# A gated-recurrence, token-mixing and gating kernel in one launch: one decay scan over all head pairs, key and query scaling on VectorE, token weights split in place by output half

## What is computed

```python
# block 1: gated linear attention, state (B, H, 48, 48)
for t in range(S):
    state = alpha[:, :, t, :, None] * state + einsum('bhd,bhe->bhde', k[:, :, t], v[:, :, t])
    y[:, :, t] = einsum('bhd,bhde->bhe', q[:, :, t], state)
# block 2, x = y as (B, S, 384)
theta = x @ w_theta
zr, zi = x * cos(theta), x * sin(theta)
y = einsum('ts,bsd->btd', w_tok_r, zr) + einsum('ts,bsd->btd', w_tok_i, zi)
u = x + y
x2 = u + maximum(u @ w_ch, 0)
# block 3
h = maximum(x2 @ w_in, 0); u, v = h[..., :512], h[..., 512:]
v_n = (v - mean(v)) / sqrt(var(v) + 1e-6)
out = (u * (einsum('ts,bsd->btd', w_spatial, v_n) + b_spatial)) @ w_out
```

## Time and profile before

| | us |
|---|---|
| median of 3 runs | 657.05 (651.57 to 658.28) |
| the profiled execution | 655.44 |
| its span, first to last instruction | 653.6 |
| PE busy | 603.7 (92%) |
| DVE busy | 408.4 (62%) |
| POOL busy | 247.4 (38%) |
| ACT busy | 224.1 (34%) |
| DMA queue of the program | 48.77 MB |
| mean granted TensorE clock | 0.963 of full speed |

### The profile page before, as it was taken

One profiled execution on the slowest core, in us unless ns is written; L12 is line 12 of the kernel. 1 busy time (PEld: TensorE's weight loads), 2 busy tenths in 40 slices (PEclk: granted clock), 3 DMA queues, 4 the chain that ended last, 5 costly groups with the idle time before them and its releaser, 6 DMA issues.

```text
span 653.6 us, 11285 instructions
## 1 busy us (share of the span) xinstructions
PE 603.7 (92%) x4608; PEld 568.1 (87%) x4608; DVE 408.4 (62%) x733; ACT 224.1 (34%) x410; POOL 247.4 (38%) x205
## 2 busy tenths in 40 slices
...
GB/s 333 164 119 109 62 62 60 62 62 97 69 55 158 62 93 66 62 155 65 50 48 105 102 48 314 2 73 0 38 36 73 1 62 12 1 1 74 0 1 73
DMA packets 18580, 49.49 MB, mean 76 GB/s; under 512 B 1632, under 2 KB 12128, under 8 KB 18016
## 3 DMA queue, kind: packets, MB, share of 16 engines
q1 hardware_dynamic: 18528, 48.77, 21.6%
...
## 4 chain that ended last, share of the span: by engine, by line
PE 61%; DVE 21%; ACT 6%; issue 5%; DMA 4%; POOL 3%; ACTq 0%; DVEq 0%
PE psY L388 10%; PE psS L487 8%; PE psF L487 8%; PE psC L370 5%; DVE akq L723 4%; PE psS L465 4%; DVE after L711 4%; PE psF L455 4%; PE psF L475 4%; PE psS L475 3%; PE psF L465 3%; DVE total L715 3%; PE psC L405 3%; PE psS L321 2%; PE psF L349 2%
## 5 line engine op out<-in xcount | busy, mean ns | idle before, releaser
L923 POOL TENSOR_TENSOR z_lo<-cos_sin,z_hi 128x768 fp32r<-128x768 f32 x24 | 46.4, 1935 | 137.0 <-ACT z_hi L579 137.0
L983 POOL TENSOR_TENSOR gated_lo<-u_gated,gated_hi 128x384 fp32r<-128x384 f32 x32 | 32.4, 1013 | 124.3 <-ACT gated_hi L675 124.2
L723 DVE TENSOR_TENSOR_SCAN akq<-akq,rtotal,zeros 128x128 f32<-128x128 f32 x96 | 56.4, 646 | 0.6
L388 PE MATMUL psY<-tok_r_hi,z_hi 128*128 128x384 f32 x144 | 52.9, 367 | 3.5 <-POOL z_lo L923 3.3
L711 DVE TENSOR_TENSOR_SCAN after<-akq,zeros 128x127 f32<-128x127 f32 x96 | 45.9, 539 | 8.8 <-DMA akq<-akq 8.8
L349 PE MATMUL psF<-v,scores 128*64 128x48 f32 x768 | 39.4, 232 | 11.1 <-issue 10.7
L388 PE MATMUL psY<-tok_i_hi,z_hi 128*128 128x384 f32 x144 | 49.1, 341 | 0.0
L388 PE MATMUL psY<-tok_r_hi,z_lo 128*128 128x384 f32 x144 | 49.1, 341 | 0.0
L388 PE MATMUL psY<-tok_i_lo,z_hi 128*128 128x384 f32 x144 | 49.0, 340 | 0.0
L388 PE MATMUL psY<-tok_r_lo,z_hi 128*128 128x384 f32 x144 | 48.9, 340 | 0.0
L388 PE MATMUL psY<-tok_i_hi,z_lo 128*128 128x384 f32 x144 | 48.8, 339 | 0.0
...
## 6 DMA issues: line engine op xcount, KB each, us to landing
...
```

Of the source, the lines that this page charges most:

```text
L388: mm = pe.matmul(psY[:, j, 0:HALF], Z[s][l][:, q, tile(j)], W[m][:, s, half(h)], start=(s == 0 and q == 0 and n == 0), stop=(s == CHUNKS - ...
L723: op = dve.tensor_tensor_scan(AKQ[s][:, 0, p, :], AKQ[s][:, 0, p, :], zeros[:], rtotal[:, s, p:p + 1], ALU.mult, ALU.add)
L923: pool.tensor_tensor(Z[c][1][:], trigs[g % 2][:], f(Z[c][0][:]), ALU.subtract).then_inc(z_lo, 1)
L983: pool.tensor_tensor(GA[1][:, j, half(h)], ug[h][:, j], f(GA[0][:, j, half(h)]), ALU.subtract).then_inc(g_lo, 1)
```

## The change

- **One scan.** The decays get a 129th column per head pair that holds 0, so that one scan over 516 columns passes from pair to pair: the tile `restart` puts a 1 there (backwards), and `rtotal`, now 517 columns with the reciprocals at every 129th, puts the pair's reciprocal there (forwards). The product over all 128 decays then stands in column 0 of each pair of `after`, so that the multiply for `total` is gone. There is one `after` instead of two.
- **Scaling on VectorE.** POOL's `scale_keys` and `scale_queries` are gone; DVE multiplies k right behind the reciprocal and q right behind the second scan.
- **Order.** In the first six chunks DVE runs `mask_scores(c)` ahead of `decay_keys(c + 1)`, and `reduce_angle(c - 1)` ahead of `decay_queries(c + 1)`; ACT runs `xT_high(c)` ahead of `sines(c - 1)`.
- **Weights.** Raw weights are loaded into the place of their low part and split there. A piece is now two row blocks by one output half (384 columns), 12 pieces as before and as large as before. `SPLITS` says behind which chunk a piece is split: the last four behind chunks 6 and 7. `w_ch` is split in chunk 4. PE's wait for everything ahead of chunk 6 is gone; it waits for the pieces of a unit, and for `ch_lo` at the first `channel_mix` (chunk 7).
- **Loads.** The decays of chunk 0 are a DMA of their own, `w_theta` is loaded ahead of chunk 1, six pieces follow, the other six behind `load_chunk(3)`.

```diff
+SEG = P + 1
+SCAN = PAIRS * SEG
+SPLITS = ((0, 1), (2, 3), (4,), (5,), (), (6, 7), (8, 9), (10, 11)) + ((),) * (BATCH * CHUNKS)
...
+        def tok_part(i):
+
+            h, rest = divmod(i, CHUNKS)
+            pair, m = divmod(rest, 2)
+            return m, slice(2 * pair, 2 * pair + 2), half(h)
...
@@ sync
             load_chunk(0)
+            sp.dma_start(raw_theta[:], w_theta.rearrange("(c p) n -> p c n", p=P)).then_inc(theta_in, 16)
             load_chunk(1)
-            sp.dma_start(raw_theta[:], w_theta.rearrange("(c p) n -> p c n", p=P)).then_inc(theta_in, 16)
-            for i in range(RAWS):
+            for i in range(CHUNKS):
                 load_tok(i)
+            load_chunk(2)
             sp.dma_start(raw_ch[:], w_ch.rearrange("(c p) n -> p c n", p=P)).then_inc(ch_in, 16)
-            for c in range(3):
-                load_chunk(2 + c)
-                load_tok(RAWS + 2 * c)
-                load_tok(RAWS + 2 * c + 1)
+            load_chunk(3)
+            for i in range(CHUNKS):
+                load_tok(CHUNKS + i)
+            load_chunk(4)
             load_chunk(5)
@@ tensor
-                if k == 0:
-                    pe.wait_ge(tok_lo, 2 * s + 2)
+                if k < HALVES:
+                    pe.wait_ge(tok_lo, k * CHUNKS + s // 2 * 2 + 2)
...
+                if n == 0:
+                    pe.wait_ge(ch_lo, 1)
...
             angles(CHUNKS - 1, 0)
-            pe.wait_ge(ch_lo, 1)
-            pe.wait_ge(tok_lo, 2 * CHUNKS)
@@ scalar
                 copy_x(c)
+                xT_high(c)
                 if c:
                     sines(c - 1)
-                xT_high(c)
                 keep_xT(c)
                 if c:
                     z_high(c - 1)
-                tok_high(2 * c)
-                tok_high(2 * c + 1)
-            act.wait_ge(ch_in, 16)
-            act.activation(WC[0][:], raw_ch[:], ACT.Copy).then_inc(ch_hi, 1)
+                if c == CHUNKS - 2:
+                    act.wait_ge(ch_in, 16)
+                    act.activation(WC[0][:], raw_ch[:], ACT.Copy).then_inc(ch_hi, 1)
+                for i in SPLITS[c]:
+                    tok_high(i)
@@ vector
-                for p in range(PAIRS):
-                    op = dve.tensor_tensor_scan(after[s][:, p, P - 2::-1], AKQ[s][:, 0, p, P - 1:0:-1],
-                                                zeros[:, 0:P - 1], 1.0, ALU.mult, ALU.add)
-                op.then_inc(after_made, 1)
+                dve.tensor_tensor_scan(after[:, ::-1], ALPHA[s][:, ::-1], restart[:, ::-1], 1.0,
+                                       ALU.mult, ALU.add).then_inc(after_made, 1)
                 dve.wait_ge(after_made, g + 1)
-                dve.tensor_tensor(total[:, s, :], after[s][:, :, 0], AKQ[s][:, 0, :, 0], ALU.mult).then_inc(total_made, 1)
-                dve.wait_ge(total_made, g + 1)
-                dve.reciprocal(rtotal[:, s, :], total[:, s, :]).then_inc(rtotal_made, 1)
+                need(dve, decayed, g)
+                dve.reciprocal(rtotal[:, 0:SCAN:SEG], AFTER[:, :, 0]).then_inc(rtotal_made, 1)
+                if g == 0:
+                    dve.wait_ge(akq_in[0], 16)
+                dve.tensor_tensor(K[s], K[s], AFTER[:, :, 1:SEG], ALU.mult).then_inc(k_scaled, 1)
...
-                for p in range(PAIRS):
-                    op = dve.tensor_tensor_scan(AKQ[s][:, 0, p, :], AKQ[s][:, 0, p, :], zeros[:],
-                                                rtotal[:, s, p:p + 1], ALU.mult, ALU.add)
-                op.then_inc(decayed, 1)
+                dve.tensor_tensor_scan(ALPHA[s], ALPHA[s], rtotal[:, 1:], rtotal[:, 0:1],
+                                       ALU.mult, ALU.add).then_inc(decayed, 1)
+                dve.wait_ge(decayed, g + 1)
+                dve.tensor_tensor(Q[s], Q[s], ALPHA[s].rearrange("p (q t) -> p q t", q=PAIRS)[:, :, 0:P],
+                                  ALU.mult).then_inc(q_scaled, 1)
...
             for c in range(CHUNKS):
+                mask_scores(c)
                 decay_keys(c + 1)
-                mask_scores(c)
-                decay_queries(c + 1)
                 if c:
                     reduce_angle(c - 1)
+                decay_queries(c + 1)
                 update_state(c)
@@ gpsimd
-            def scale_keys(g):
-                pool.wait_ge(after_made, g + 1)
-                pool.tensor_tensor(AKQ[g % 2][:, 1], AKQ[g % 2][:, 1], after[g % 2][:], ALU.mult).then_inc(k_scaled, 1)
-
-            def scale_queries(g):
-                pool.wait_ge(decayed, g + 1)
-                pool.tensor_tensor(AKQ[g % 2][:, 2], AKQ[g % 2][:, 2], AKQ[g % 2][:, 0], ALU.mult).then_inc(q_scaled, 1)
...
             for c in range(CHUNKS):
-                scale_keys(c + 1)
-                scale_queries(c + 1)
                 if c:
                     z_low(c - 1)
-                tok_low(2 * c)
-                tok_low(2 * c + 1)
-            pool.wait_ge(ch_hi, 1)
-            pool.tensor_tensor(WC[1][:], raw_ch[:], f(WC[0][:]), ALU.subtract).then_inc(ch_lo, 1)
+                if c == CHUNKS - 2:
+                    pool.wait_ge(ch_hi, 1)
+                    pool.tensor_tensor(WC[1][:], raw_ch[:], f(WC[0][:]), ALU.subtract).then_inc(ch_lo, 1)
+                for i in SPLITS[c]:
+                    tok_low(i)
```

More of the change, by code:

```diff
@@ L108, in build @@
         work_at = r.offset
-        AKQ = [r(f"akq{i}", [3, PAIRS, P]) for i in range(2)]
+        AKQ = [r(f"akq{i}", [SCAN + 2 * PAIRS * P]) for i in range(2)]
         late_at = r.offset
-        after = [r(f"after{i}", [PAIRS, P]) for i in range(2)]
+        after = r("after", [SCAN])
         V = [r(f"v{i}", [D]) for i in range(2)]
```

118 lines of the change are left out of this document (63 added, 55 removed).

## The result

| | us |
|---|---|
| changed kernel, median of 4 runs | 635.13 (634.82 to 635.71) |
| before, 4 runs on the same chip | 655.87 (651.57 to 658.28) |
| ratio, 95% interval | 0.9692 [0.9638, 0.9746] |
| profiled execution's span, before and after | 653.6, 633.0 |

The change saves 20.7 us; the profiled spans differ by 20.6. The forecast was 645.0, a saving of 11.3 in the profile.

What follows compares the result with a forecast made beforehand. PE bounds 115.14 to 350.00 us; in early chunks DVE waits for POOL, and PE idles ahead of chunk 6. Terms -1.8 - 1.8 + 0.3 - 1.5 - 8.0 + 0.6 + 0.9 = -11.3 from 655.44; forecast 645.0 us, range 637 to 652.

Steps and rivals of the forecast that it cites:

- the start: Start and chunks 0 and 1: chunk 0's scores start earlier and `update_state(1)` ends at 29.1 instead of 30.9, -1.8 us.
- chunk 5 with the gate: Chunk 5's angles no longer wait for `xT_lo`, -1.5 us; PE's wait ahead of chunk 6 goes, -7.96 us.
- rival 3: Steady chunks: a long scan costs far more than four short ones; loses from 1.86 us, up to 664 us; chance 0.07.
- Rival 1: Only removing PE's wait ahead of chunk 6 pays, early chunks keep their 15 us: 647.4 us; chance 0.19.
- Rival 4: Chunks 6 to 8 give back 4 to 6 us more, the last pieces sharing POOL: about 650 us; chance 0.11.
- Rival 2: Early chunks gain more if the clock stays at 2.4 GHz: chunk 4 some 14 us, about 639 us; chance 0.13.
- Chunk 2: DVE's chain meets POOL's work, the scan just missing the door: 14.9 us against 14.5 before.
- Chunk 4: PE's own 16.7 us, which it keeps, as DVE's lead doesn't help: +0.3 us.
- Chunk 6: `z_lo(5)` is late behind POOL's pieces 6 and 7, PE idle some 3 us: +0.6 us.
- Chunks 7 and 8: They carry pieces 8 to 11, POOL's `u_lows` come behind 8 and 9, `L769` held once more: +0.6 and +0.3 us.
- Steady chunks and the rest: 17 steady chunks to 350 us: DVE's chain behind `z_lo` 2.67 against 2.66 us, sum 0; bounds -2.5 to +20 us.
- 17 x 0.16 us: Steady chunks: one long scan might hold `z_lo` off, +2.7 us instead of 0; the rows were said to favour 0.

Runs made afterwards that it cites:

- the filled gaps: Changed kernel with 12 matmuls whose result nobody uses added behind `transpose_x` of chunks 1 to 3: 631.87 us, ratio 0.9636.

## Why the prediction was right in direction and too small

Right: the start (-1.7 against -1.8), chunk 3, and chunk 5 with the gate (-9.5 both). The durations of the new instructions came out as estimated (scan 1.23 to 1.28 us against 1.2, multiply 0.69 against 0.71), so rival 3 fell. Rival 1 fell too: the stretches up to the end of chunk 4 gained 6.8 us besides the gate. Rival 4 did not come about: chunk 7 gave back 0.2 us. Rival 2 is nearest, but only part of what it named happened: chunks 2 and 3 took 12.7 and 12.8 us (it had 12.5), yet at clocks of 0.80 and 0.77 and not at the full one, and chunk 4 took 15.7 and not 14.

Five terms of the sum failed, all to the same side:

- **Chunk 2, "14.9 us", since "the scan just misses the door"**: 12.74. The scan met `z_lo`'s end. 2.2 us.
- **Chunk 4, "PE's own 16.7 us and keeps them"**: -1.0, 1.3 us from +0.3. PE nearly full at a clock of 0.77 is not PE's own time; the window is 0.81 now. Length times granted clock is nearly the same wherever it was read: 12.9 us before (16.70 x 0.77), 12.7 in the changed kernel (15.74 x 0.81), 12.8 with the queries on POOL (14.59 x 0.88) and 13.1 with the filled gaps (13.06 x 1.00).
- **Chunk 6, "+0.6"**: -1.35, 1.9 us. I priced the turn as a wait removed and `z_lo(5)` late, with some 3 us of idle time of PE. The row of before holds a clock of 0.81 behind the gate, and this went with the gate and the pieces spread out: now it is 1.00, and 0.78 with both put back (15.4 us). `z_lo(5)` was late by 0.98 us only, since L798 fell between the pieces.
- **Chunks 7 and 8, "+0.6 and +0.3"**: +0.2 to the mask of chunk 8 and nothing seen behind it, 0.7 us.
- **Steady chunks and the rest, "at most 2.5 us can be won", 0 taken**: -2.7 to chunk 23 and -0.5 behind it, 3.2 us (the -0.5 is block 3, within what it varies by). The bound was read from PE's idle time, which leaves out the 0.16 us by which every wait hides under the last matmul's drain. My chain of 2.66 against 2.67 us measured to the end of the last query instruction; to `xT_lo`, which counts, it is 2.58 against 2.40. With the queries on POOL the same stretch takes 205.0 us, 4.8 less than before: that much there was to win.

Together 2.2 + 1.3 + 1.9 + 0.7 + 3.2 = 9.3, the 9.3 us between -11.3 and -20.6.

The low clock is in two of the terms, chunks 4 and 6, where PE is nearly full and its time follows the clock. All windows of chunks 2 to 4 together tell how long PE stood at 1.2 GHz, as twice the missing share times the length. Before: 2 x 0.34 x 14.51 + 2 x 0.31 x 15.16 + 2 x 0.23 x 16.70 = 26.9 us; after: 2 x 0.20 x 12.74 + 2 x 0.23 x 12.82 + 2 x 0.19 x 15.74 = 17.0 us. That this cost anything in chunk 2 isn't shown: with the filled gaps it took the same time at the full clock. There the gain is DVE's, which passes POOL's pieces with fewer instructions.

One error went the other way and was hidden by these. The forecast had both multiplies in DVE's chains (0.71 us each) and gave POOL's two scalings no worth, since "`q` was never late". It never asked what the kernel takes without the query multiply on DVE. The run that puts it back on POOL is 7.9 us faster: in its trace 5.1 us before the mask of chunk 8, where PE waits for the state behind that multiply, and only 2.1 in the steady stretch, where PE has no more than the holes to give. The rest of the change is thus worth more than the 20.7 us, and this part gave some 8 of it back.

By the Trainium skill, page "SBUF — State Buffer", section "Who interferes with whom", whichever engine issues first holds the shared pair for its instruction. The rows agree: the POOL piece behind the scan, which had started first, took 2.75 us instead of 1.8. The cost feared from it, 17 x 0.16 us, did not appear: steady `z_lo` takes 1.84 us behind the long scan and 1.97 behind four short ones.

What each part is worth, from the runs that undo it (each uncertain by some 3 us, as said above): one scan for four 7.9, `total` 3.4, gate and spread weights 8.5, orders 4.5, scaling moved to DVE -7.9 to -8.4. They sum to some 16 of 20.7 us. The parts aren't additive (the gate is worth 3.9 alone), and the early loads and the place of the raw weights were not run apart, so the other 5 us stay undivided.
